# Attention windows, a gated mixture and a wide MLP in one kernel: probabilities scaled before the turn, and five smaller moves

## What is computed

```python
# attention: B, H, S, D = 2, 8, 768, 64; a key is kept if it is one of the first 8,
# or at most 95 positions behind the query
scores = q @ k.T / sqrt(D) - slope[h] * dist        # kept keys only
a = exp(scores - max(scores))
a = a / (sum(a) + 1e-9)
x = a @ v                                           # -> [1536, 512]
# mixture: four experts, F = 1024
p = domain_probs / (domain_probs.sum(-1) + 1e-9)
out = sum over e of p[:, e] * (relu(x @ w1[e]) @ w2[e])
# gated MLP
h = (out @ w1b) * (out @ w2b) @ w3
y = h @ w_out                                       # [1536, 512]
```

## Time and profile before

| | us |
|---|---|
| median of three runs | 843.34 |
| the profiled execution | 843.51 |
| its span in the trace | 841.5 |
| TensorE busy | 828.4 (98%) |
| GpSimd busy | 529.9 (63%) |
| VectorE busy | 401.5 (48%) |
| ScalarE busy | 324.8 (39%) |

### The profile page before, as it was taken

One profiled execution on the slowest core, in us unless ns is written; L12 is line 12 of the kernel. 1 busy time (PEld: TensorE's weight loads), 2 busy tenths in 40 slices (PEclk: granted clock), 3 DMA queues, 4 the chain that ended last, 5 costly groups with the idle time before them and its releaser, 6 DMA issues.

```text
span 841.5 us, 13307 instructions
## 1 busy us (share of the span) xinstructions
PE 828.4 (98%) x4974; PEld 784.0 (93%) x4974; DVE 401.5 (48%) x902; ACT 324.8 (39%) x627; POOL 529.9 (63%) x466
## 2 busy tenths in 40 slices
PE   9999998999999999999999999999999999999998
PEld 8777777999999999999899899999999999999987
DVE  6755565541533633634766436136246245266520
ACT  4566575341521531532343445224224134234411
POOL 3556567477666556558487697846836836938920
PEclk9999999999999999999999999999999999999999
DMA  8833542232221221221034133223113123101202
GB/s 334 332 102 113 170 136 102 77 113 76 93 77 51 95 76 51 96 74 51 25 126 126 65 104 122 80 69 100 51 69 100 51 69 101 51 26 51 84 19 78
DMA packets 25365, 79.62 MB, mean 95 GB/s; under 512 B 3264, under 2 KB 4560, under 8 KB 25296
## 3 DMA queue, kind: packets, MB, share of 16 engines
q1 hardware_dynamic: 21200, 70.68, 24.7%
q10 hardware_dynamic: 4032, 8.00, 2.7%
q0 software_dynamic: 64, 0.03, 0.0%
HBM read 71.85 MB, written 6.84 MB: 94 GB/s over the span
## 4 chain that ended last, share of the span: by engine, by line
PE 75%; POOL 11%; issue 5%; DVE 4%; ACT 2%; DMA 1%; SPq 0%; DVEq 0%; ACTq 0%; POOLq 0%
PE bank L50 23%; PE bank L52 23%; PE bank L51 23%; PE bank L576 3%; POOL al L1005 2%; POOL al L1015 2%; PE bank L593 2%; PE bank L564 2%; POOL diag L472 1%; ACT ah L991 1%; POOL bl L1074 1%; POOL a_sum L973 1%; POOL a_sum L980 1%; POOL a_sum L971 1%; POOL raw L978 1%
## 5 line engine op out<-in xcount | busy, mean ns | idle before, releaser
L50 PE MATMUL bank<-bh,ah 128*128 128x384 f32 x672 | 226.0, 336 | 3.8 <-DVE parts L1498 1.8
L52 PE MATMUL bank<-bh,al 128*128 128x384 f32 x672 | 224.6, 334 | 0.0
L51 PE MATMUL bank<-bl,ah 128*128 128x384 f32 x672 | 224.6, 334 | 0.0
L50 PE MATMUL bank<-hh,w2h 128*128 128x384 f32 x512 | 171.0, 334 | 0.0
L51 PE MATMUL bank<-hl,w2h 128*128 128x384 f32 x512 | 171.0, 334 | 0.0
L52 PE MATMUL bank<-hh,w2l 128*128 128x384 f32 x512 | 171.0, 334 | 0.0
L1005 POOL TENSOR_TENSOR al<-a_sum,ah 128x768 fp32r<-128x768 f32 x48 | 88.7, 1849 | 94.5 <-ACT ah L991 94.5
L1028 POOL TENSOR_TENSOR w2l<-raw,w2h 128x1024 fp32r<-128x1024 f32 x40 | 96.1, 2409 | 80.3 <-ACT w2h L1023 79.7
L50 PEld LDWEIGHTS bank<-bh,ah 128*128 128x128 f32 x672 | 126.1, 188 | 7.8 <-DVE parts L1498 3.4
L51 PEld LDWEIGHTS bank<-bl,ah 128*128 128x128 f32 x672 | 126.2, 188 | 0.1
L52 PEld LDWEIGHTS bank<-bh,al 128*128 128x128 f32 x672 | 126.2, 188 | 0.0
(11 more groups left out here) (111 smaller groups left out, 1220.1 us busy)
## 6 DMA issues: line engine op xcount, KB each, us to landing
raw<-weights SPq DMA_DIRECT2D x80, 512.0 KB, 3.4
k<-k SPq DMA_DIRECT2D x8, 704.0 KB, 7.2
v<-v SPq DMA_DIRECT2D x8, 704.0 KB, 4.5
raw<-folded SPq DMA_DIRECT2D x8, 512.0 KB, 3.9
fold_mt_raw<-m3t SPq DMA_DIRECT2D x7, 512.0 KB, 9.2
q<-q SPq DMA_DIRECT2D x8, 384.0 KB, 5.6
out<-rows ACTq DMA_DIRECT2D x11, 256.0 KB, 2.0
gate<-gates ACTq DMA_DIRECT2D x7, 384.0 KB, 4.0
```

The costliest lines, as they stand in the source:

```text
L50: nc.tensor.matmul(out, wh, xh, start=start, stop=False, skip_group_check=adds_on)
L51: nc.tensor.matmul(out, wh, xl, start=False, stop=False, skip_group_check=adds_on)
L52: return nc.tensor.matmul(out, wl, xh, start=False, stop=stop, skip_group_check=adds_on)
```

## The change

- `turn_over` uses TensorE's transpose against the identity instead of a product with a diagonal. GpSimd multiplies the probabilities themselves by the reciprocals, in place and before the turn (128x512 elements a unit where `diag` had 128x256); the buffers `diag` go, and so does GpSimd's wait for `turned`.
- VectorE makes sum and reciprocal of couple c+2 in turn c (before: c+1), behind `outputs` instead of ahead of it, and waits for the exponentials of the same turn.
- In the dense stage the subtraction that overwrites raw quarter a21 is second of the four sums; ScalarE rounds the raw quarters as soon as that is done, ahead of the sums, and GpSimd makes the raw quarters' low parts ahead of the sums'.
- The first two pieces of `w_out` are issued from ScalarE's queue, at the head of its list, instead of from SyncE's.
- In `gated`, `product5` of the second group goes ahead of `product6` of the first, and `product2` of the second ahead of `product7` of the first; no product is left between `product7` and `product4` of the first group.
- In the attention's last turns the splits are placed anew: B21's high part in turn 17 instead of 14, B22's in turn 22 instead of 16, and the low parts of B22 and T4 are made by VectorE behind its loop instead of by GpSimd in turns 21 and 22.

```diff
@@ Fold.first_loads, Fold.scalar
             sp.dma_start(self.mt_raw[0][:, c], self.m3t[0][:, c]).then_inc(self.first_loaded[s], 16)
-            wo(s)
...
     def scalar(self, act):
+        for s in range(2):
+            c = self.half(s)
+            act.dma_start(self.wo_raw[:, c], self.m_out[:, c]).then_inc(self.wo_loaded[s], 16)
@@ WindowAttention.gpsimd
                 pool.wait_ge(self.inverted, u // 2 + 1)
-                if u >= 2:
-                    pool.wait_ge(self.turned, u - 1)
-                ident = self.setup.ident[:, :].rearrange("p (h k) -> p h k", h=1).to_broadcast([P, 2, P])
-                scale = self.rden[u // 2 % (NS // 2)][:, r:r + 2].rearrange("p (h k) -> p h k", k=1).to_broadcast([P, 2, P])
-                self.nc.gpsimd.tensor_tensor(self.diag[u % 2][:, :].rearrange("p (h k) -> p h k", h=2), ident, scale,
-                                             ALU.mult).then_inc(self.spread, 1)
+                probs = self.pr[u % NS][:, 0:2 * w].rearrange("p (h k) -> p h k", h=2)
+                scale = self.rden[u // 2 % (NS // 2)][:, r:r + 2].rearrange("p (h k) -> p h k", k=1).to_broadcast([P, 2, w])
+                self.nc.gpsimd.tensor_tensor(probs, probs, scale, ALU.mult).then_inc(self.normed, 1)
@@ WindowAttention.vector
-        if 0 <= u + 2 < UNITS:
-            den = self.den[(c + 1) % (NS // 2)][:, :]
-            dve.wait_ge(self.exped, u + 4)
-            nc.vector.tensor_scalar(den, den, 1e-9, None, ALU.add).then_inc(self.summed, 1)
-            dve.wait_ge(self.summed, c + 2)
-            nc.vector.reciprocal(self.rden[(c + 1) % (NS // 2)][:, :], den).then_inc(self.inverted, 1)
         if 0 <= u < UNITS and (u + 2) % PER_OUT == 0:
             self.outputs(dve, u // PER_OUT)
+        if 0 <= u + 4 < UNITS:
+            den = self.den[(c + 2) % (NS // 2)][:, :]
+            dve.wait_ge(self.exped, u + 6)
+            nc.vector.tensor_scalar(den, den, 1e-9, None, ALU.add).then_inc(self.summed, 1)
+            dve.wait_ge(self.summed, c + 3)
+            nc.vector.reciprocal(self.rden[(c + 2) % (NS // 2)][:, :], den).then_inc(self.inverted, 1)
@@ WindowAttention.turn_over
-            last = self.nc.tensor.matmul(self.ps_t[u % 2][:, cols], self.pr[u % NS][:, cols],
-                                         self.diag[u % 2][:, head * P:(head + 1) * P], start=True, stop=True)
+            last = self.nc.tensor.transpose(self.ps_t[u % 2][:, cols], self.pr[u % NS][:, cols],
+                                            self.setup.ident[:, :])
@@ Dense.up_sums, up_high, up_raw_high, up_low
         nc.gpsimd.tensor_tensor(s1, a21, a22, ALU.add).then_inc(self.a_step, 1)
         pool.wait_ge(self.a_step, 4 * g + 1)
+        nc.gpsimd.tensor_tensor(a21, a11, a21, ALU.subtract).then_inc(self.a_step, 1)
         nc.gpsimd.tensor_tensor(s2, s1, a11, ALU.subtract).then_inc(self.a_step, 1)
...
     def up_high(self, act, g):
+        if g >= 3:
+            act.wait_ge(self.p3, g - 2)
+        self.up_raw_high(act, g)
         self.up_sums_high(act, g)
-        self.up_raw_high(act, g)
...
     def up_raw_high(self, act, g):
         nc, s = self.nc, self.slot(g)
+        act.wait_ge(self.a_step, 4 * g + 2)
...
     def up_low(self, pool, g):
+        self.up_raw_low(pool, g)
         self.up_sums_low(pool, g)
-        self.up_raw_low(pool, g)
@@ Dense.gated
         self.product1(pe, i0 + 1)
+        self.product5(pe, i0 + 1)
         self.product6(pe, i0)
-        self.product5(pe, i0 + 1)
+        self.product2(pe, i0 + 1)
         self.product7(pe, i0)
-        self.product2(pe, i0 + 1)
         self.product4(pe, i0)
@@ build, the vector block, behind the loop over turns
+                dense.b_split_low(dve, nc.vector, T4, 0)
+                dense.b_split_low(dve, nc.vector, B22, 0)
                 dense.vector(dve)
```

More of the change, by code:

```diff
@@ L426, in __init__ @@
         self.pt = [sb(f"pt{s}", [P, 2 * WIN]) for s in range(2)]
-        self.diag = [at_high(nc, f"diag{s}", [P, 2 * P]) for s in range(2)]
         self.ps_s, self.ps_t, self.ps_o = bank[0:4], bank[4:6], bank[6]
@@ L435, in __init__ @@
         self.inverted = sem("inverted")
-        self.spread = sem("spread")
+        self.normed = sem("normed")
         self.turned = sem("turned")
@@ L465, in gpsimd @@
             if 0 <= u < UNITS:
[L466 removed]
+                w, r = self.width(u), u % 2 * 2
                 pool.wait_ge(self.inverted, u // 2 + 1)
[L468 to L473 removed]
+                probs = self.pr[u % NS][:, 0:2 * w].rearrange("p (h k) -> p h k", h=2)
+                scale = self.rden[u // 2 % (NS // 2)][:, r:r + 2].rearrange("p (h k) -> p h k", k=1).to_broadcast([P, 2, w])
+                self.nc.gpsimd.tensor_tensor(probs, probs, scale, ALU.mult).then_inc(self.normed, 1)
     def exponentials(self, act, u):
@@ L568, in turn_over @@
     def turn_over(self, pe, u):
-        pe.wait_ge(self.spread, u + 1)
+        pe.wait_ge(self.normed, u + 1)
         if u >= 2:
             pe.wait_ge(self.odd_copied if u % 2 else self.even_copied, u // 2)
-        tiles = self.width(u) // P
-        for m in range(2 * tiles):
-            cols, head = slice(m * P, (m + 1) * P), m // tiles
-            last = self.nc.tensor.matmul(self.ps_t[u % 2][:, cols], self.pr[u % NS][:, cols],
-                                         self.diag[u % 2][:, head * P:(head + 1) * P], start=True, stop=True)
+        for m in range(2 * self.width(u) // P):
+            cols = slice(m * P, (m + 1) * P)
+            last = self.nc.tensor.transpose(self.ps_t[u % 2][:, cols], self.pr[u % NS][:, cols],
+                                            self.setup.ident[:, :])
         last.then_inc(self.turned, 1)
@@ L955, in slot @@
         return (g + 2) % 3
-    def up_sums(self, pool, g):
-        self.up_sums12(pool, g)
-        self.up_sums34(pool, g)
     def up_quarters(self, g):
@@ L963, in up_quarters, with up_sums @@
         return [t[:, q * QUART:(q + 1) * QUART] for t, q in ((raw, 0), (raw, 1), (raw, 2), (raw, 3), (s, 0), (s, 1), (s, 2))]
-    def up_sums12(self, pool, g):
+    def up_sums(self, pool, g):
         nc = self.nc
@@ L1757, in _ @@
                         dense.up_raw_high(act, c // 4)
-                    if folded_by < c < folded_by + 5:
-                        dense.b_split_high(act, SPLITS[c - folded_by], 0)
+                    if c == folded_by + 1:
+                        dense.b_split_high(act, T1, 0)
+                    if c == folded_by + 3:
+                        dense.b_split_high(act, T2, 0)
+                    if c == folded_by + 5:
+                        dense.b_split_high(act, B21, 0)
                     if c == folded_by + 7:
@@ L1763, in _ @@
                         dense.b_split_high(act, T4, 0)
+                    if c == folded_by + 10:
+                        dense.b_split_high(act, B22, 0)
                     windows.copy_even(act, c)
@@ L1820, in _ @@
                         dense.b_split_low(pool, nc.gpsimd, T3, 0)
-                    if c == folded_by + 9:
-                        dense.b_split_low(pool, nc.gpsimd, B22, 0)
-                    if c == folded_by + 10:
-                        dense.b_split_low(pool, nc.gpsimd, T4, 0)
                 dense.gpsimd(pool)
@@ L1829, in _ @@
                 full.gpsimd(pool)
-                for b in SPLITS:
+                for b in (B11, T1, B21, T2, T3):
                     dense.b_split_low(pool, nc.gpsimd, b, 0)
```

9 lines of the change are left out of this document (1 added, 8 removed).

## The result

The changed kernel takes 832.98 us (median of 4 runs, 832.21 to 833.77), the kernel before 843.75 (843.16 to 844.31): a ratio of 0.987, 95% interval 0.986 to 0.989. I had forecast 837.5 with a range of 829 to 846. Sign and range held; the gain was 10.8 us where I had counted 6. The profiled execution took 832.98 with a span of 830.7.

A forecast was written before the change was run, and what follows sets the result against it. TensorE was taken to bound the kernel, busy 828.4 of 841.5 us. From 843.5, attention gains 3.9, VectorE's low parts lose 0.2 and the dense stage gains 2.1: 837.7, or 837.5 as median; range 829 to 846.

The forecast's parts named there:

- The second rival: Attention: transposes as dear as the products they replace (0.248 us), time about 843; chance 0.10.
- Transposes: TensorE's turn over: 0.11 us a tile instead of 0.248, a wide turn over falling from 1.98 to 0.88.
- Scaling: GpSimd in the attention: 1.25 us for each 128x512 scaling, bounds about 1.23 to 1.32.
- The hold of the small sum: VectorE in the attention: small sum held until GpSimd's current operation ends, 0.6 to 1.2 us a turn, bounds 0 and 1.82.
- my first rival: Attention: small sum hardly held, window stage gains about 11 us, time 830.5; chance 0.25.
- Turns: Attention turn by turn: start loses 1.5, turns 2-11 gain 5.5, 12 loses 0.9, 13-20 lose 1.4, 21-23 gain 2.2.
- Dense stage: Dense stage: 2.1 us gained from raw quarters first and the new gated order together, bounds 0.5 and 3.
- Raw first: Dense stage: raw quarters first shortens GpSimd's loop from 8.2 to 7.3 and removes three TensorE idle places, gaining 1.8 us.
- the order: Gated stages: new product order removes a 0.8 us idle place, adds a wait behind `product7`, gains 0.3 for both.
- First loads: Start of the kernel: two queues gain zero, up to 0.3 us either way, hidden behind VectorE's first window.
- last low parts: End of the attention: low parts of T4 and B22 on VectorE lose 0.2 us, at most 1.5.
- The clock: Attention turns without fold: TensorE's clock falls to 1.2 GHz, attend and scores double, time 858; chance 0.10.

The follow-up runs named there:

- experiment 2: Changed kernel with an ordinary product against the identity in place of each TensorE transpose: 843.91 us.
- experiment 3: Changed kernel with a small GpSimd multiplication (128x32, result unused) added behind each scaling: 837.0 us.
- Experiment 1: Changed kernel without VectorE's small sum, the addition of 1e-9 ahead of the reciprocal: 827.85 us.
- experiment 12: Kernel of Experiment 1 (no addition of 1e-9) with the sums of T2, T3 and T4 moved from GpSimd to VectorE: 829.89 us.
- experiment 6: Changed kernel with the gated stages' products in the order of the kernel before: 832.98 us.
- Experiments 5: Changed kernel with its first loads in SyncE's queue alone, as before the change: 832.56 us.
- 11: Changed kernel with the low parts of T4 and B22 back on GpSimd in turns 21 and 22: 832.40 us.
- experiment 7: Changed kernel with sums ahead of raw quarters again in the dense stage, on ScalarE and GpSimd: 838.13 us.
- experiment 4: Changed kernel with three extra unused 128x128 products in each of TensorE's idle places of turns 12 to 14: 832.61 us.
- experiments 8: Changed kernel with the reciprocal back where it was, for the next couple and first in VectorE's turn: 832.24 us.
- 9: Changed kernel with the reciprocal back for the next couple, first in VectorE's turn, and without the addition of 1e-9: 829.46 us.
- 10: Changed kernel with sums ahead of raw quarters and the old order of the gated stages together: 837.5 us.

## Why the prediction was right, and where it was off

**The frame held.** TensorE was the chain in turns with fold steps, and its shorter turn over was the gain: experiment 2 gives back all of it. The second rival had put such a kernel at 843; it measured 843.9. In the changed kernel the chain of these turns runs also over ScalarE's exponentials and VectorE's sums and biases, as the odd turns and the store turns of the forecast had it.

**Transposes, 0.11 a tile (0.057 to 0.248).** Measured 0.128 (8 in 1.02). My way to it, the load of 128 columns as twice the 55 ns between the two rows, came out close; the load's mean is 144 ns, and no run shows that it is the load that sets the rate. The Trainium skill's "4× faster for FP32" (page "TensorE: Matmul & The Clock Gate", Terms) would have given 0.062 of the 0.248 that a product took; this trace shows 1.9 times faster.

**Scaling, 1.25.** This was the mis-sized term. Its mean is 1.04 and two take 2.04. I had set its lower end at twice the 0.614 of a 128x256 operation, "or some less since a part of each is fixed", and then took a value above that end. The new rows have both sizes, 0.614 and 1.040, so 256 columns more cost 0.43 and 0.19 is fixed. Through the loop in turns 13 to 20 this gives 0.4 of a turn, and experiment 3, which puts the 0.2 back into each scaling, brings 4.40 against my 4.5 and 837.0 against my 837.5. That the totals agree so well is partly chance: 1.4 of its 3.8 were lost ahead of turn 13, nearly all of it ahead of the first scaling.

**The hold of the small sum, 0.6 to 1.2 a turn (0 to 1.82).** The mechanism was right and was seen from two rows. The mean hold was 0.494 - 0.158 = 0.34, with single ones up to 1.9. In turns 2 to 11 the ten sums between 50 and 97 us were held for 3.5 together, where my five odd turns with 0.6 had 3.0. Experiment 1 prices it at 5.1 us for 24 sums, 0.2 each, the sum itself and its hold together. At 833.0 the kernel lies between the forecast (837.5) and my first rival, sums hardly held (830.5), a little nearer to the rival. The Trainium skill, page "GPSIMD Engine Reference", Key points, puts such contention down to shared SBUF interfaces with VectorE's 2-port modes and two-SBUF-input instructions. The rows of experiment 12, with two SBUF inputs, agree. The small sum has one, and no row shows its mode; the reciprocal, the copies and the biases are free of the hold in the rows.

**Turns.** Turn 2 at 51.3 (50.61), turn 12 at 97.4 (96.78): the loss at the start and the gain of the fold turns were within 0.7. The mean of turns 2 to 11 is 4.62, exactly mine, but by luck: five odd turns of 4.6, five even ones of 4.35 and 2 for the stores make 4.68, not 4.62. The shorter narrow turns aren't among these terms, and a wide even turn takes 4.50 (88.00 to 92.50). Turns 13 to 20, which I had losing 1.4, gained 1.8 (8 x 0.23). That makes 3.2 of the 4.0 by which the attention ended ahead of the forecast.

**Dense stage, 2.1.** Measured 2.9. The three idle places went and the one behind `product7` came, as written. Raw first I had put at 1.8, with a loop of 7.3 a group (measured 7.52); the order at 0.3, and it is 0 (experiment 6). From the last odd `attend` to the last idle place of the first gated stage (before from 148.30 to 419.34, after from 140.44 to 411.44) the time is unchanged, 271.0; the gain lies behind that. So raw first carries this gain, and the mis-sized term is the price of an idle place, for which I had 0.6: against the same products in experiment 6, the kernel before loses 0.8, 0.7 and 0.9 at its three. I didn't foresee that the additions' new order makes GpSimd's loop longer, which only shows when raw first is undone.

**First loads, 0; last low parts, -0.2.** Experiments 5 and 11 don't contradict either, and can't tell them from 0.4 or 0.6 the other way. That VectorE's first window hides what TensorE does at the start held in the changed kernel's profile (32.64 against 32.60) and not in those of experiments 3 and 7, where the window came at 33.86 and 33.66 and waited for TensorE's scores.

**The clock.** I gave it 0.10 and argued that no gap of TensorE reaches 2 us. The argument failed: the clock fell at 103 behind gaps of 0.96 and 1.02 that came close together. What I had wrong in the rival as well was its price: it doubled `attend` and scores and charged it all to the turn, where the scores went from 1.13 to 1.88, and 0.6 of the 1.6 us arrived at the end (experiment 4). The Trainium skill (same page on TensorE, Part 4) says that transposes don't count as busy; here turns whose TensorE work is one third transposes kept 1.00 from 108 to 140, and no run separated that rule from plain idleness.

## What to carry to other kernels

When an engine's work is cut, price the loop that takes over with the new operation's own fixed and per-column parts: two rows of different sizes give both, and 0.2 us in a twice-a-turn operation was worth some 2.7 to 4 us here (experiment 3). A tiny VectorE operation can be the dearest of the turn if it is of a kind that is held beside GpSimd; look at least, median and greatest of its duration, not at the median, and try to leave it out before moving work around it. A change of order can be worth nothing for one neighbour and much for another: measure each part undone by itself.

## What the hardware showed that I had not expected

- **The hold takes either side, and not the same in every execution.** VectorE's tables at the start run beside a GpSimd low tile. In the changed kernel's profile the row of VectorE was held (2.62 instead of 0.42) and the tile passed; in the profile of experiment 7, the same code up to there, all of VectorE's rows of that line stayed at 0.42 and the tile took 4.57 (4.64 in experiment 3):

```profile
25.43 2.54 POOL L204 TENSOR_TENSOR fold_mt_l<-fold_mt_raw,fold_mt_h 128x1024 fp32r<-128x1024 f32 x1 [2.98 <-ACT fold_mt_h L155]
...
25.63 2.62 DVE L378 SCALAR_TENSOR_TENSOR bias_w<-bias_tmp,bias_tmp 128x256 f32<-128x256 f32 x1
```

```profile
26.47 4.57 POOL L204 TENSOR_TENSOR fold_mt_l<-fold_mt_raw,fold_mt_h 128x1024 fp32r<-128x1024 f32 x1 [2.92 <-ACT fold_mt_h L155]
```

  The next low tile began at 33.88 instead of 32.85 there, and turn 1 about 1.0 later (45.79 against 44.77). But the hold isn't where that 1.0 comes from: the low tile itself began at 26.47 instead of 25.43, and the one before it at 21.02 instead of 19.99. What the longer tile did was to keep TensorE waiting for 0.42 at 31.09.
- **The lateness begins with the first products.** TensorE's first product of the fold, in the changed kernel's profile and then in that of experiment 7:

```profile
6.95 0.47 PE L50 MATMUL bank<-fold_wo_h,fold_mt_h 128*128 128x512 f32 x1 [1.76 <-DVE fold_wo_l L199]
```

```profile
6.96 0.77 PE L50 MATMUL bank<-fold_wo_h,fold_mt_h 128*128 128x512 f32 x1 [0.83 <-DVE fold_wo_l L199]
```

  The next products start 0.43 apart up to 10.51 in experiment 7, and 0.23 apart in the changed kernel, though the granted clock reads 1.00 in both. Experiment 3's profile has the same. No run shows the cause; it may be part of the 1.5 us by which the runs of one kernel differ.
- **The same idle pattern of TensorE was followed by a fall of the clock in one profile and not in another** (the changed kernel's and experiment 6's). Falls as long as that one also stood in the profiles of experiments 8, 9, 10 and 12, each behind some us in which TensorE was busy 0.13 to 0.66; the kernel before, whose TensorE had no such stretch there, shows none.
- **A transpose of a 128x128 float32 tile is one instruction of 0.128 us, start to start; the product with an identity in its place is two and takes 0.248.**
